# Expert results scattered into expert order with their token numbers, a second network that takes them in that order, and outputs scattered to their tokens by POOL

## The reference, cut to what matters

```python
# 1. gated linear attention, 4 batches x 8 heads x 768 steps x 48
state = alpha[:, :, t, :, None] * state + einsum('bhd,bhe->bhde', k[:, :, t], v[:, :, t])
y[:, :, t] = einsum('bhd,bhde->bhe', q[:, :, t], state)
x = y.transpose(0, 2, 1, 3).reshape(3072, 384)

# 2. mixture of 8 experts, each token goes to the one with the highest logit
logits = normalized(x) @ normalized(expert_emb).T / tau
e = argmax(logits); gate = softmax(logits)[e]
x[mask] = gate[mask, None] * (maximum(x[mask] @ w1[e], 0) @ w2[e])     # 384 -> 1024 -> 384

# 3. the second network, the same weights for every token
h = x @ w_in                          # 384 -> 2048
out = maximum(0.01 * h, h) @ w_out    # 2048 -> 384
```

## Time and profile before

| | |
|---|---|
| time of three runs, us | 863.32, 863.24, 861.77; median 863.24 |
| the profiled execution's own time, us | 862.47 |
| its span, first to last instruction, us | 860.5 |
| PE busy | 841.3 us (98% of the span) |
| PEld, DVE, ACT, POOL busy | 88%, 49%, 40%, 19% |
| mean granted TensorE clock | 0.994 of full speed |
| chain that ended last | PE 93%, DVE 3%, DMA 1%, POOL 1% |

### The profile page before, as it was taken

How to read it: one execution, slowest core, us unless ns; L and a number is a source line. 1 busy time by engine, 2 the same in 40 slices (tenths; PEclk the granted TensorE clock), 3 DMA queues, 4 the chain that set the end, 5 groups by cost and what they waited for, 6 DMA issues and landing times.

```text
span 860.5 us, 17386 instructions
## 1 busy us (share of the span) xinstructions
PE 841.3 (98%) x5580; PEld 758.7 (88%) x5581; DVE 417.7 (49%) x640; ACT 342.9 (40%) x663; POOL 160.3 (19%) x210
## 2 busy tenths in 40 slices
PE   8999999999999999999969999999999999999998
PEld 7888888999999999999958999998999999999997
DVE  7998968525543525454254433433443443343332
ACT  3555556533543535434233323333333333333323
POOL 6766616222222232223110000000000000000000
PEclk9999999999999999999998999999999999999999
DMA  9999753625344234435031003002001100000101
GB/s 224 255 216 221 182 174 110 219 69 183 119 150 150 104 110 155 145 107 191 10 71 41 1 0 74 2 1 73 0 0 42 31 0 14 24 0 1 37 1 37
DMA packets 45266, 76.25 MB, mean 89 GB/s; under 512 B 16231, under 2 KB 35731, under 8 KB 45232
## 3 DMA queue, kind: packets, MB, share of 16 engines
q1 hardware_dynamic: 41104, 64.97, 27.1%
q0 software_dynamic: 3968, 10.82, 3.7%
q10 hardware_dynamic: 160, 0.01, 0.0%
HBM read 61.63 MB, written 15.53 MB: 90 GB/s over the span
## 4 chain that ended last, share of the span: by engine, by line
PE 93%; DVE 3%; DMA 1%; POOL 1%; issue 1%; ACT 0%; SPq 0%; POOLq 0%; DVEq 0%; ACTq 0%
PE bank L1416 24%; PE bank L1423 24%; PE bank L1366 15%; PE bank L1346 15%; PE bank L1357 3%; PE bank L1190 3%; PE bank L1230 2%; PE bank L1207 2%; PE bank L1238 1%; PE bank L1333 1%; PE bank L1196 1%; PE bank L1181 1%; PE bank L1250 1%; DMA yl<-y_rows 1%; POOL kt L541 0%
## 5 line engine op out<-in xcount | busy, mean ns | idle before, releaser
L1416 PE MATMUL bank<-yT,wts 128*128 128x512 f32 x864 | 217.9, 397 | 6.8 <-DVE yT L1139 6.8
L1423 PE MATMUL bank<-wts,gs 128*128 128x384 f32 x1152 | 217.3, 337 | 0.0
L1423 PEld LDWEIGHTS bank<-wts,gs 128*128 128x128 f32 x1152 | 204.5, 188 | 8.9 <-issue 0.4
L1416 PEld LDWEIGHTS bank<-yT,wts 128*128 128x128 f32 x864 | 162.6, 190 | 37.5 <-DVE yT L1139 7.6
L1157 DVE TENSOR_TENSOR g<-bank,small 128x512 f32<-128x512 f32 x96 | 66.5, 693 | 181.2 <-ACT small L788 181.2
L1346 PE MATMUL bank<-wts,gxT 128*128 (+1 forms) x558 | 141.5, 398 | 0.6 <-DVE gxT L1079 0.6
L1366 PE MATMUL bank<-wts,hT 128*128 x744 | 137.3, 339 | 1.5 <-DVE hT L1110 1.5
L788 ACT ACTIVATE small<-bank 128x512 f32<-128x512 f32 x96 | 57.5, 599 | 191.7 <-PE bank L1416 191.6
L1366 PEld LDWEIGHTS bank<-wts,hT 128*128 128x128 f32 x744 | 128.5, 188 | 1.9 <-issue 1.8
L1346 PEld LDWEIGHTS bank<-wts,gxT 128*128 128x128 f32 x558 | 101.9, 188 | 19.8 <-issue 0.8
L1159 DVE TENSOR_TENSOR gs<-g,gs 128x512 fp32r<-128x512 f32 x96 | 66.5, 693 | 67.1 <-ACT gs L791 67.1
(11 more groups left out here) (166 smaller groups left out, 702.2 us busy)
## 6 DMA issues: line engine op xcount, KB each, us to landing
raw<-w SPq DMA_DIRECT2D x14, 1536.0 KB, 7.0
qkas<-qka SPq DMA_DIRECT2D x40, 289.5 KB, 5.2
vs<-v SPq DMA_DIRECT2D x24, 192.0 KB, 4.7
x_rows<-xs SPq DMA_DIRECT2D x24, 192.0 KB, 4.3
yl<-y_rows SPq DMA_DIRECT2D x24, 192.0 KB, 4.5
out<-os SPq DMA_DIRECT2D x5, 768.0 KB, 4.3
raw<-w_in SPq DMA_DIRECT2D x2, 1536.0 KB, 7.0
raw<-w_out SPq DMA_DIRECT2D x2, 1536.0 KB, 7.3
```

The costliest lines, as they stand in the source:

```text
L1416: m = pe.matmul(gps[f % 2][:, :], wts[:, 0, w_part, n:n + P], yT[:, u, y_part, k], start=(k == 0 and (w_part, y_part) == (0, 0)), stop=(k ...
L1423: m = pe.matmul(ops[tt], gs[:, f % 4, g_part, tt * P:(tt + 1) * P], wts[:, 1, w_part, f * D:(f + 1) * D], start=(f == 0 and (g_part, w_par ...
```

## The change

Rows of the second network now stand in expert order. Routing makes `slot_dst` not from the token number but from the place: the place (`slot_row`, a constant from a new iota) less the number of filled-up places ahead of it (`more` summed over the experts before). Rows of `y_dram` are 388 numbers wide: 384 of data and four behind, of which the first is the token number, which POOL copies from `slot_src` into `ys` before each scatter. Because the first 512 sorted rows are complete once window 10 is scattered, `load_y` of the first two groups waits for windows 10 and 14 alone and stands ahead of w_out's loads in SP's queue. The turning and splitting of group 0 moves into window 29 on DVE and ACT. `inner(0, 0, 0)` moves into window 30 on PE, between `turn_h` and `contract`; the 26 unused matmuls go; the second half of w_out's split moves into slices 2 to 4 of group 0. POOL scatters each 128 finished rows of `os` to their tokens' rows of `out` by an indirect DMA, with token numbers that SP loads from the last columns of `y_dram` when all windows are scattered; SP no longer stores. To have `yT`, `os` and the windows' tiles alive together, `small`, `g` and `gs` are laid over tiles of the windows. ACT's and DVE's loops over pairs of groups are written out; PE's stays a hardware loop.

```diff
-    y_blk = y_dram.rearrange("(g n r) (j d) -> g j r n d", r=SQ, j=QUADS, n=GT // SQ)
+    y_blk = y_dram[:, 0:D].rearrange("(g n r) (j d) -> g j r n d", r=SQ, j=QUADS, n=GT // SQ)
+    y_token = y_dram[:, D:YW].rearrange("(t p) d -> p t d", p=P)
...
+            def load_y(t, u):
+                newest = min(t * TG + TG - 1 + E - 1, WINDOWS - 1)
+                for j in range(2):
+                    sp.wait_ge(scattered[j], 16 * ((newest + 2 - j) // 2))
+                if t >= 2:
+                    sp.wait_ge(yt_turned, (t - 1) * KD)
+                for j in range(QUADS):
+                    sp.dma_start(yl[j * SQ:(j + 1) * SQ, u],
+                                 y_blk[t:t + 1, j].rearrange("a r n d -> (a r) n d")).then_inc(yl_in[u], 16)
+            load_y(0, 0)
+            load_y(1, 1)
             for half in range(2):
                 sp.wait_ge(w_lo, SET_IN * PIECES + 3 * half + 3)
                 load_half(half, w_out[half * F:(half + 1) * F].rearrange("(k p) n -> p k n", p=P))
             for j in range(2):
                 sp.wait_ge(scattered[j], 16 * ((WINDOWS + 1 - j) // 2))
-            load_y(0, 0)
-            load_y(0, 1)
...
+            sp.dma_start(tokens[:, :, :], y_token).then_inc(tokens_in, 16)
+            for t in range(2, GROUPS):
+                load_y(t, t % 2)
...
+            pool.iota(slot_row[:, :], [[P, WINDOWS]], base=0, channel_multiplier=1,
+                      allow_small_or_imprecise_dtypes=True).then_inc(consts_made, 1)
...
-            pool.wait_ge(tables_ready, 2)
+            pool.memset(ys[:, :, D:YW], 0.0).then_inc(id_space, 1)
             pool.wait_ge(gx_turned, 1)
             gather(0, slot_src[:, 2:3])
+            pool.wait_ge(id_space, 1)
+            pool.wait_ge(tables_ready, 3)
...
                 wait_scattered(pool, w, u, pool_turns)
+                pool.tensor_copy(ys[:, u, D:D + 1].bitcast(I32), slot_src[:, ds(w, 1)]).then_inc(idx_copied, 1)
...
+            pool.wait_ge(tokens_in, 16)
+            for t in range(GROUPS):
+                for tt in range(TG):
+                    n = t * TG + tt
+                    pool.wait_ge(o_copied, n + 1)
+                    pool.indirect_dma_start(
+                        out=out, out_offset=bass.IndirectOffsetOnAxis(ap=tokens[:, n, 0:1].bitcast(U32), axis=0),
+                        in_=os_[:, t % 2, tt], in_offset=None, bounds_check=N - 1, oob_is_err=False).then_inc(stored[t % 2], 16)
...
+                if nxt and not nxt2:
+                    for k in range(KD):
+                        y_round(0, 0, k)
...
-            act.wait_ge(ye_ready, WINDOWS + 1)
-            split_hi(act, SET_OUT, 1, W2_PIECES)
...
+                        if t == 0 and 2 <= f < 2 + len(W2_PIECES):
+                            act.wait_ge(ye_ready, WINDOWS + 1)
+                            split_hi(act, SET_OUT, 1, W2_PIECES[f - 2:f - 1])
...
-            start("side", dve.tensor_tensor(far, clear, empty, ALU.add))
-            after("side")
-            dve.wait_ge(tables_ready, 1)
-            dve.tensor_copy(slot_dst[:, :], far).then_inc(tables_ready, 1)
...
+            start("main", dve.tensor_tensor(wexp[:, :, 0:E - 1], wexp[:, :, 0:E - 1],
+                                            more.unsqueeze(1).to_broadcast([P, W, E - 1]), ALU.mult))
+            after("main")
+            start("main", dve.tensor_reduce(far, wexp[:, :, 0:E - 1], AX.X, ALU.add))
+            after("main")
+            start("main", dve.tensor_tensor(far, slot_row[:, :], far, ALU.subtract))
+            after("main")
+            start("main", dve.tensor_tensor(far, far, empty, ALU.add))
+            after("main")
+            dve.wait_ge(tables_ready, 2)
+            dve.tensor_copy(slot_dst[:, :], far).then_inc(tables_ready, 1)
...
-            split_lo(dve, SET_OUT, 1, W2_PIECES)
             dve.sem_inc(g_done, 2)
...
+                if not nxt:
+                    pe.wait_ge(w_lo, SET_IN * PIECES + 3)
+                    inner(0, 0, 0)
                 pe.wait_ge(w_lo, e * PIECES + PIECES)
...
                 contract(w, u, par)
...
-            pe.wait_ge(w_lo, (SET_IN + 1) * PIECES)
-            keep_busy(Y_BUSY, gps[1][:, :], wts[:, 0, 0, 0:P], wts[:, 0, 0, 0:GT])
-            inner(0, 0, 0)
             inner(0, 0, 1)
-            pe.wait_ge(w_lo, (SET_OUT + 1) * PIECES)
+            pe.wait_ge(ys_ready, WINDOWS)
+            pe.wait_ge(w_lo, SET_OUT * PIECES + 3)
```

More of the change, by code:

```diff
@@ L474, in _ @@
                 sp.wait_ge(scattered[j], 16 * ((WINDOWS + 1 - j) // 2))
[L476 to L480, removed]
-            load_y(0, 0)
-            load_y(0, 1)
[L485 to L501, removed]
-            groups(GROUPS // 2 - 1, True)
-            for u, s in enumerate(stored):
-                sp.wait_ge(s, 16 * (GROUPS // 2 + 1 + u * (TG - 1)))
+            sp.dma_start(tokens[:, :, :], y_token).then_inc(tokens_in, 16)
+            for t in range(2, GROUPS):
+                load_y(t, t % 2)
         @block.gpsimd
@@ L722, in _, with y_round @@
             relu(0, 0, 1)
[L723 removed]
+            act.wait_ge(tables_ready, 2)
+            def y_round(t, u, k):
+                act.wait_ge(yt_turned, t * KD + k + 1)
+                act.activation(yT[:, u, 0, k], yf[:, (u * KD + k) % 2], ACT.Copy).then_inc(yt_hi, 1)
             def step(w, u, nxt, nxt2):
@@ L1038, in _ @@
             tok, clear, empty, far, ghi = (slot_val[:, j, :] for j in range(5))
+            more = exp8[:, 6, 0:E - 1]
+            start("side", dve.tensor_tensor(more, base[:, 1:E], base[:, 0:E - 1], ALU.subtract))
             dve.wait_ge(slots_summed, 1)
@@ L1117, in step @@
                     split_lo(dve, e, par, W2_PIECES)
+                if nxt and not nxt2:
+                    y_turn(0, 0, 0)
+                    y_turn(0, 0, 1)
+                    y_rest(0, 0, 0)
+                    dve.wait_ge(yt_lo, 1)
+                    y_turn(0, 0, 2)
+                    y_rest(0, 0, 1)
+                    y_rest(0, 0, 2)
                 if not nxt:
@@ L1165, in groups @@
                             y_turn(t + 1, 1 - u, f - Y_FROM)
-            with dve.Fori(0, GROUPS // 2 - 1) as i:
-                groups(i, False)
-            groups(GROUPS // 2 - 1, True)
+                        if t == 0 and 2 <= f < 2 + len(W2_PIECES):
+                            split_lo(dve, SET_OUT, 1, W2_PIECES[f - 2:f - 1])
+            for i in range(GROUPS // 2):
+                groups(i, i == GROUPS // 2 - 1)
         @block.tensor
@@ L1376, in _, with inner @@
             hidden(0, 0, 0, 1)
-            pe.wait_ge(tables_ready, 3)
+            pe.wait_ge(tables_ready, 2)
+            def inner(t, u, f):
+                if f == 0 and not isinstance(t, int):
+                    pe.wait_ge(yt_lo, t * KD + KD)
+                s = t * FT + f
+                if not (isinstance(t, int) and t == 0 and f < 2):
+                    pe.wait_ge(g_done, s + 1)
+                if f == FT // 2:
+                    pe.wait_ge(w_lo, (SET_IN + 1) * PIECES)
+                for k in range(KD):
+                    if f == 0 and isinstance(t, int):
+                        pe.wait_ge(yt_lo, t * KD + k + 1)
+                    for w_part, y_part in PARTS:
+                        n = f * P // F * 3 * PC + k * F + f * P % F
+                        m = pe.matmul(gps[f % 2][:, :], wts[:, 0, w_part, n:n + P], yT[:, u, y_part, k],
+                                      start=(k == 0 and (w_part, y_part) == (0, 0)), stop=(k == KD - 1 and w_part == 1))
+                m.then_inc(g_ready, 1)
             def step(w, u, nxt, nxt2):
@@ L1401, in _ @@
             each_window(pe, step)
-            def inner(t, u, f):
-                if f == 0 and not isinstance(t, int):
-                    pe.wait_ge(yt_lo, t * KD + KD)
-                s = t * FT + f
-                if not (isinstance(t, int) and t == 0 and f < 2):
-                    pe.wait_ge(g_done, s + 1)
-                for k in range(KD):
-                    if f == 0 and isinstance(t, int):
-                        pe.wait_ge(yt_lo, t * KD + k + 1)
-                    for w_part, y_part in PARTS:
-                        n = f * P // F * 3 * PC + k * F + f * P % F
-                        m = pe.matmul(gps[f % 2][:, :], wts[:, 0, w_part, n:n + P], yT[:, u, y_part, k],
-                                      start=(k == 0 and (w_part, y_part) == (0, 0)), stop=(k == KD - 1 and w_part == 1))
-                m.then_inc(g_ready, 1)
             def add_rows(u, f, tt):
```

105 lines of the change are left out of this document (45 added, 60 removed).

## The result

| | before | changed |
|---|---|---|
| median, us (of the kernel before one run more than in the section above) | 862.55 (861.77 to 863.32, 4 runs) | 855.61 (854.18 to 856.75, 4 runs) |
| ratio to before | 1 | 0.9919, 95% [0.9897, 0.9941] |
| profiled execution, its own time / span, us | 862.47 / 860.5 | 856.75 / 855.0 |

The changed kernel is faster by 7.0 us (0.0081 of 862.55; interval 5.1 to 8.9), where 14.5 were forecast. Its time lies above the range given.

A forecast was written before the change was run, and what follows sets the result against it. PE, busy 98% of the span, was taken as the bound, with one pause at the handover. -17.4 + 2.7 + 0.1 + 0.1 = -14.5 from 862.47 gave 848.0 us, range 845.4 to 852.1.

The forecast's parts named there:

- The end: After the last matmul: POOL's four queued scatters replace SP's stores, 2.7 us more; bounds 1.1 and 5.0 more.
- rival: A pause stays, 854 us, 0.08; third group late, 865 at a 102 us load, 0.03; gap not closed, 862 to 865, 0.03.
- the handover: From the end of window 30's turn_h, less 1.54, to the first outward: 27.99 us becomes 10.53, so 17.4 go.
- the 1.54 wait: Ahead of window 30's product, PE waits for DVE's rest of the hidden rows; 1.54 us, to go.
- 0.28 of the longer product: Window 30's product was 0.28 us longer than window 29's; this was to go.
- the pause and the low clock: Behind the last window's product: 12.7 us of pause and 3.05 of low clock, both to go.
- The possible wait of 0.1: Before inner(0,0,2), PE might wait for slice 0's activation: 2.16 us against 2.08 of cover, taken as 0.1.
- Start and routing: Before window 0: one more iota and five later DVE steps; 0.1 us each, bounds 0 to 0.2 and 0 to 0.5.
- Windows: POOL copies one more column per window and scattered rows are longer; both covered by POOL's waiting and buffer slack.
- The token numbers' load, the rival: Before group 2's rows on SP's queue: a slow load delays the second network, 865 us if it takes 102; chance 0.03.
- The 6 us: Token numbers' load: 192 pieces per DMA engine at 29 ns each, if size plays no part, take 6 us.

The follow-up runs named there:

- first run: The changed kernel with its block ended without POOL's drain; POOL still waits for all output scatters: 846.93 us, ratio 0.9809.
- third: The changed kernel with an extra POOL drain after the windows' scatters and token load, ahead of the output scatters: 851.26 us, ratio 0.9854.
- second: The changed kernel with the last group's rows stored by SP as plain stores, left in expert order: 845.02 us, ratio 0.9781.
- the run before it: The changed kernel with only inner(0, 0, 0) put back behind the last window's product; early loads and turning stay: 858.13 us, ratio 0.9929.

## Why the prediction was wrong

**What failed is the paragraph "The end".** It counted what POOL issues and when the last scatter lands, +2.7, with +5.0 as the upper bound. That part was right to 0.1: 5.14 us from the last matmul to POOL's last landing, where the kernel before needs 2.49 (SP sees its last store land at 860.1, and the last matmul ends at 857.61), so +2.6. But it took the landing for the end of the program, and so put what POOL does behind it at nothing; the section on the change says likewise that the end hangs on POOL's last scatter. POOL then drains for 7.1 us, and the true term is +9.75. The trace of before held this cost, in POOL's queue under the line that closes the program, and the chain of waits passes it at 441.10; I read only what PE waited for there. No rival named it either: each was about the handover or the loads of the second network, and none of them happened. Leaving the drain out (first run) shortens the end by 7.1 us, and paying most of it early (third) by 5.0 (from 12.64 to 7.63), in each case the part of the drain that goes from the end. Hiding it (second) shortens the end by 9.8, the drain and the +2.6 of the queue together.

**The handover was right, and so were its parts.** Forecast -17.4, in the profiles -17.5: the 1.54 wait and 0.28 of the longer product come back as 1.9 when slice 0 is undone; of the pause and the low clock, 5.1 come back when the turning is undone, and 10.5 are left to the kernel before. The possible wait of 0.1 behind the last window did not occur. What the prediction could not know is that the profiled execution of before had the dearest handover: from the end of window 29's product to the first `outward` it is 28.87 there, and 28.01, 27.83 and 27.35 in the three others (with 9.12, 8.58 and 7.96 us for the 27 matmuls at the low clock, where the earlier trace rows has 9.29). These 27 matmuls in the chains of the three:

```profile
452.98 9.12 PE bank L1416 x27
```

```profile
454.40 8.58 PE bank L1416 x27
```

```profile
456.84 7.96 PE bank L1416 x27
```

The changed kernel has 11.35 in each of its three. So 16.7 is the mean gain, not 17.4.

**The sum with the drain put in.** -16.7 + 2.6 + 7.1 = -7.0, and the 0.7 between the first `outward` and the last matmul: -7.7. The prediction had put this stretch at nothing. The 0.7 belongs to the change, since the stretch is 395.9 us in all four profiles of the kernel before and 395.2 in all three of the changed kernel; no cause was sought. The two measurements are -7.0 (5.1 to 8.9) and -8.5 (6.5 to 10.6). Without the drain it would be -14.8, and the first run gave 0.0191 of 863.99, -16.5 (14.2 to 18.8). So only one term of any size was missing.

**The smaller terms.** Start and routing, +0.1 each: not to be seen, as the means of 150.69 and 150.74 show. Windows no longer than before: 284.17 us in both. The token numbers' load, the rival that was to cost time from 86 us on and make the kernel slower than before over 100, lands in 3.6, as the DMA view says:

```profile
tokens<-y_rows SPq DMA_DIRECT2D x1, 48.0 KB, 3.6
```

The 6 us that the prediction worked out from the pieces in the pause were too high: 192 pieces for each DMA engine in 3.6 us are 19 ns each at most, where those of 384 bytes had taken 29, so the 16-byte pieces were not the slower ones. POOL's wait for the new `slot_dst` was 6.8 us once, ahead of the fourth window's gather, as the prediction had it (from 145 to 151), and the windows took no longer.

The estimate for one scatter by the Trainium skill, "DMA: Bandwidth & Descriptors", section "Anatomy of one DMA — SWDGE (gpsimd) path", 2.45 us, is near the 2.6 from 844.88 to 847.5; as the prediction held against it, four of them make a queue. Another page says where the landing must not be read: by the Trainium skill, "Perfetto Trace Analysis", section "DMA Instruction — SWDGE (GPSIMD)", the profiler's end of such an instruction is when its descriptors are made, not when the data have moved. The trace agrees in that the last one ends at 845.86, and POOL's wait for the landing only 1.6 us later.

## What to carry to other kernels

When a change makes an engine the last to finish, price what that engine does after its last piece of work as well: read its sequencer's rows at the line that closes the program, which in the kernel before may lie hundreds of microseconds ahead of the end and cost nothing there. On POOL this is a drain whose length grows with the DMAs that it has issued. Let another engine do the last stores (shown here only with a kernel that leaves its last rows in expert order), or drain once beside other work, or end the block without it where the program itself waits for every store. Of the kernels that do the whole work, the two without it are the fastest, 0.9809 and 0.9822 of the kernel before and not told apart. The first of them is faster than the changed kernel by 7.1 us of span.

## What the runs showed of the hardware that was not expected

- POOL's drain takes 0.083 us for each indirect DMA issued since the last drain, though all of them have landed: 2.01 us after 24, 5.14 after 62, 6.77 after 82, 7.10 after 86. Whether it counts DMAs, their 128 rows or their bytes was not told apart. The drains of the other engines at the same line are of another kind: in the changed kernel DVE's takes 0.73 us, ACT's 0.52 and that of PE's weight queue 3.34, and each ends where the engine's last instruction ends (838.83, 842.9 and 842.34, the instructions 838.82, 842.88 and 842.36), so they add nothing; SP's takes 0.12. POOL's runs on for 7.10 us when nothing of POOL's is left. The Trainium skill, "VectorE: DVE Perf Modes", section "The DRAIN you can't avoid", tells the pipeline flush behind each VectorE instruction from boilerplate drains in the preamble and postamble, about 12 ns each on all engines; POOL's drain at the end of the block, at 7.10 us, fits neither.
- In the run with group 0 turned behind the windows, PE did 1.0 us of work between 440 and 444, and behind that the granted clock was 0.50 for 3 us, the lower of its two levels, which cost 1.8 us. Behind the wait of 1.64 us in the run before it, the granted clock was 1.00.
- Up to window 0 one and the same program varies by 4.6 us between executions (148.66 to 153.25; 2.3 of it between two on one chip), which in the first two single profiles looked like an effect of the change.
- A plain store by SP at the end, 1.9 us from issue to landing in the first profile of the kernel before, took 4.1 once in its second profile (least 1.9, median 2.1).
